# The up products of two MLPs by Strassen's seven half-size products, and attention written out without loops

## The chip, the cores and the metric

The kernel runs on one core of one Trainium2 chip. The metric is device time in microseconds (us) of one launch, lower being better. The kernel before takes 647.9 us, the median of 3 runs (647.8 to 647.93).

## What is computed

The program is an attention block followed by two MLPs. Everything is float32; matrices are multiplied as two float32r parts (a high part and the rest, "hi" and "lo"), three products each: hi·hi, lo·hi and hi·lo.

```
scores = q @ k.T / sqrt(D) + bias(head, distance)      # B=2, H=8, S=768, D=64
keep   = key < n_global  or  0 <= query - key < n_local  # 8 and 96
x  = softmax(where(keep, scores, -1e9)) @ v               # -> 1536 tokens x 512
h  = x @ w_in1;  x2 = (h * sigmoid(h)) @ w_out1           # 512 -> 2048 -> 512
h2 = x2 @ w_in2; y  = (h2 * clip(h2+3, 0, 6) / 6) @ w_out2
```

## The kernel before

**Attention** goes over 8 pairs of heads, 6 query tiles of 128 each: 48 units u. Since a query sees the last 96 keys and 8 global ones, a unit takes 256 columns of keys. For each unit TensorE (PE) makes the scores (L747), turns the probabilities (L756) and multiplies them by the values (L766); VectorE (DVE) adds the bias and finds the row maximum (L427), ScalarE (ACT) makes the exponentials (L596), GpSimd (POOL) normalizes (L301), DVE and ACT share the copies of the turned probabilities (L439, L614), and every third unit ACT and DVE split a group of 384 output columns into `x_hi` and `x_lo` (L619, L444). The pairs run in loops over two pairs (`pairs`), the first and last turn written out.

**The MLPs** work on blocks of 384 tokens (`TB`; `NBLK` = 4 blocks) and chunks of 128 units of the inner width (`FC` = 16). For a chunk PE runs `up` (L849): 4 parts of the depth times 3 terms, 12 matmuls of 384 columns into one of four PSUM banks. In the first MLP ACT takes the sigmoid (L635) and DVE multiplies (L413); in the second DVE does both steps (L566, L570). ACT rounds to `g_hi` (L679), DVE takes the rest, `g_lo` (L542, L575). Then comes `down1` (L864, 12 matmuls of 384 columns) or, in the second MLP, `down2` (L878, 9 matmuls of 512 columns). The order on PE is written by hand: `up` runs two chunks (`AHEAD`) ahead of `down`.

```
for fc in range(FC):
    nxt = fc + AHEAD
    ...
        up(c + AHEAD, FC * mlp + nxt, tb, nxt)
    ...
    down(c, tb, fc, first, last and mlp == 1 and fc == FC - 1)
```

**Weights** stay in SBUF. Each chunk of both matrices (128x1024 in all) comes once per MLP into one of three staging buffers, ACT rounds it to `w_hi` (L641), POOL takes the rest, `w_lo` (L343); both parts then serve all four blocks. Each engine has its own program; the order on each is the order of the code, and semaphores hold it back. SP only issues DMAs.

Of the kernel before, what the change touches and what calls it, by code (L numbers as in the profile page):

```python
# [19 lines left out]
FC = DF // P  # L33
TB = 384
NBLK = NB * S // TB
# [8 lines left out]
STAGES = 3  # L44
LAG = 4
DEEP = 6
AHEAD = 2
# [9 lines left out]
def build(nc, qT, kT, v, w_in1, w_out1, w_in2, w_out2, n_glob, n_loc, out):  # L57
    outer = ExitStack()
    with outer:
# [5 lines left out]

        x_hi = sb("x_hi", [P, 2, NB * KT, TB], F32R)
        x_lo = sb("x_lo", [P, 2, NB * KT, TB], F32R)

        HEAD = 4
        wa_hi = sb("wa_hi", [P, HEAD, 1024], F32R)
        wa_lo = sb("wa_lo", [P, HEAD, 1024], F32R)
        wstage = sb("wstage", [P, STAGES, 1024])
# [5 lines left out]


        attn = ExitStack()
        with attn:
# [3 lines left out]
            with ExitStack() as banded:  # L87
# [12 lines left out]
                m_bias = sb("m_bias", [P, 2, MW], F32, banded)  # L100
                m_tmp = [sb(f"m_tmp{i}", [P, MW], F32, banded) for i in range(5)]
# [10 lines left out]


        gate = sb("gate", [P, 2, TB])
        g_f = sb("g_f", [P, 2, TB])
        g_hi = sb("g_hi", [P, 2, TB], F32R)
        g_lo = sb("g_lo", [P, 2, TB], F32R)
        wb_hi = sb("wb_hi", [P, FC - HEAD, 1024], F32R)
        wb_lo = sb("wb_lo", [P, FC - HEAD, 1024], F32R)
        y_out = sb("y_out", [P, HALF, DM])  # L120
# [5 lines left out]
        def y_bank(i): return ps[:, i, :]  # L126
        def h_bank(c): return ps[:, 4 + c % 4, 0:TB]

        def w_hi(fc): return wa_hi[:, fc, :] if fc < HEAD else wb_hi[:, fc - HEAD, :]
        def w_lo(fc): return wa_lo[:, fc, :] if fc < HEAD else wb_lo[:, fc - HEAD, :]  # L130

        def x_slot(x, it, half):

            return x[:, half, bass.ds(it, 1), :].rearrange("p a t -> p (a t)")

        def x_group(x, j, gm):

# [19 lines left out]
        x_hi_ok = sem("x_hi_ok"); x_lo_ok = sem("x_lo_ok")  # L157
        w_raw = [sem(f"w_raw{i}") for i in range(STAGES)]
        w_hi_ok = sem("w_hi_ok"); w_lo_ok = sem("w_lo_ok")
        h_done = sem("h_done"); gate_ok = sem("gate_ok")  # L160
        g_ok = sem("g_ok"); g_hi_ok = sem("g_hi_ok"); g_lo_ok = sem("g_lo_ok")
        down_done = sem("down_done"); y_hi_ok = sem("y_hi_ok"); y_lo_ok = sem("y_lo_ok")
        relu_ok = sem("relu_ok")
# [3 lines left out]
        a_prt_ok = sem("a_prt_ok"); a_pv = sem("a_pv"); a_xhi = sem("a_xhi"); a_xlo = sem("a_xlo")  # L167
        dve_turn = sem("dve_turn"); pool_turn = sem("pool_turn"); sp_turn = sem("sp_turn")
        y_tile = sem("y_tile"); y_copied = sem("y_copied"); stored = sem("stored")
# [776 lines left out]
```

## Time and profile before

| | |
|---|---|
| median of 3 runs | 647.9 us |
| the profiled execution's own time | 647.83 us |
| its span | 646.1 us |
| PE busy | 627.8 us, 97% |
| DVE / ACT / POOL busy | 260.7 / 208.5 / 128.2 us |
| moved by DMA | 33.16 MB |

The profile is of one execution. Its span runs from the first instruction to the last; the execution's own time is 1.7 us longer. The page gives busy time per engine, the span in 40 slices of about 16 us, and the chain of waits that ended last. A matmul's record lasts until its results are out, so matmuls overlap: the rate is the distance from start to start, not the duration.

### The profile page before, as it was taken

Reading aid. Unit: us, or ns where it says so; the run is one execution under the profiler, and the core shown is the slowest. Engines: PE = TensorE matmul, PEld = TensorE weight load, DVE = VectorE, ACT = ScalarE, POOL = GpSimd, SP = SyncE. Lnnn points to the kernel's source line nnn. Section 1 sums busy time; section 2 is a strip of 40 time slices with the busy share of each in tenths; the row PEclk is TensorE's granted clock in tenths of the full one; section 3 lists DMA queues with packets and bytes.
Section 4 is the critical chain, followed back from the end, with each engine's and each line's share of the span. In section 5 each row is a group of like instructions: output and inputs, shape, how many; then the busy total and the mean of one; then the engine's idle time right before and its main releaser. Section 6 shows DMA issues by size and latency. Waiting matters only on the chain.

```text
span 646.1 us, 10234 instructions
## 1 busy us (share of the span) xinstructions
PE 627.8 (97%) x3600; PEld 566.4 (88%) x3600; DVE 260.7 (40%) x658; ACT 208.5 (32%) x483; POOL 128.2 (20%) x191
## 2 busy tenths in 40 slices
PE   3999998999999999999999999999999999999997
PEld 1555666999999999999999999999999999998996
DVE  4677794322332223222322253443343443343442
ACT  2777875443322223222444431112111111111112
POOL 2656666653000000000255540000000000000000
PEclk9999999999999999999999999999999999999999
DMA  5253643443000000000033300001000100001001
GB/s 197 70 183 112 223 143 132 131 131 97 1 1 2 0 1 0 0 0 0 33 131 125 112 25 0 1 1 49 2 1 0 50 0 0 0 1 50 0 1 49
DMA packets 14872, 33.16 MB, mean 51 GB/s; under 512 B 1904, under 2 KB 2160, under 8 KB 14832
## 3 DMA queue, kind: packets, MB, share of 16 engines
q1 hardware_dynamic: 14832, 32.65, 14.8%
q8 instruction: 23, 0.38, 0.2%
q14 instruction: 17, 0.14, 0.1%
HBM read 29.49 MB, written 3.15 MB: 51 GB/s over the span
## 4 chain that ended last, share of the span: by engine, by line
PE 91%; DVE 3%; issue 2%; ACT 2%; DMA 1%; DVEq 0%; ACTq 0%; POOL 0%; SPq 0%; POOLq 0%
PE ps L849 42%; PE ps L864 21%; PE ps L878 21%; PE ps L747 3%; PE ps L766 3%; PE ps L756 2%; ACT probs L596 1%; DVE negs L427 1%; DMA words<-in_n_loc 1%; DVE probsT L439 1%; ACT m_bias L604 0%; ACT x_hi L619 0%; DVE x_lo L444 0%; DVE g_lo L542 0%; DVE negmax L427 0%
## 5 line engine op out<-in xcount | busy, mean ns | idle before, releaser
L679 ACT ACTIVATE g_hi<-g_f 128x384 fp32r<-128x384 f32 x128 | 67.2, 525 | 332.1 <-PE ps L878 220.2
L849 PE MATMUL ps<-x_hi,wb_hi 128*128 128x384 f32 (+1 forms) x384 | 130.1, 339 | 0.0
L849 PE MATMUL ps<-x_lo,wb_hi 128*128 128x384 f32 (+1 forms) x384 | 130.0, 339 | 0.0
L849 PE MATMUL ps<-x_hi,wb_lo 128*128 128x384 f32 (+1 forms) x384 | 129.8, 338 | 0.0
L542 DVE TENSOR_TENSOR g_lo<-g_f,g_hi 128x384 fp32r<-128x384 f32 x64 | 37.1, 579 | 102.3 <-ACT g_hi L679 99.6
L575 DVE SCALAR_TENSOR_TENSOR g_lo<-g_f,g_hi 128x384 fp32r<-128x384 f32 x64 | 36.4, 568 | 98.1 <-ACT g_hi L679 98.1
L849 PEld LDWEIGHTS ps<-x_hi,wb_hi 128*128 128x128 f32 x384 | 72.0, 188 | 2.1
L849 PEld LDWEIGHTS ps<-x_hi,wb_lo 128*128 128x128 f32 x384 | 72.1, 188 | 2.0
L849 PEld LDWEIGHTS ps<-x_lo,wb_hi 128*128 128x128 f32 x384 | 72.1, 188 | 0.0
L413 DVE TENSOR_TENSOR g_f<-ps,gate 128x384 f32<-128x384 f32 x64 | 35.6, 556 | 84.9 <-ACT gate L635 84.9
L343 POOL TENSOR_TENSOR wb_lo<-wstage,wb_hi 128x1024 fp32r<-128x1024 f32 x24 | 58.1, 2424 | 45.6 <-ACT wb_hi L641 45.5
L864 PE MATMUL ps<-g_hi,wb_hi 128*128 128x384 f32 x192 | 64.8, 338 | 0.0
L864 PE MATMUL ps<-g_hi,wb_lo 128*128 128x384 f32 x192 | 64.6, 336 | 0.0
L864 PE MATMUL ps<-g_lo,wb_hi 128*128 128x384 f32 x192 | 64.4, 336 | 0.0
L566 DVE TENSOR_SCALAR gate<-ps 128x384 f32<-128x384 f32 x64 | 35.7, 557 | 59.4 <-PE ps L849 59.4
L878 PE MATMUL ps<-wb_lo,g_hi 128*128 128x512 f32 x144 | 56.9, 395 | 0.0
L878 PE MATMUL ps<-wb_hi,g_hi 128*128 128x512 f32 x144 | 56.7, 394 | 0.0
L878 PE MATMUL ps<-wb_hi,g_lo 128*128 128x512 f32 x144 | 56.2, 390 | 0.0
L635 ACT ACTIVATE gate<-ps 128x384 f32<-128x384 f32 x64 | 31.4, 491 | 66.5 <-PE ps L849 66.4
L596 ACT ACTIVATE probs<-negs,negmax 128x256 f32<-128x256 f32 (+1 forms) x96 | 46.3, 483 | 18.1 <-DVE negmax L427 17.3
L343 POOL TENSOR_TENSOR wa_lo<-wstage,wa_hi 128x1024 fp32r<-128x1024 f32 x6 | 14.3, 2388 | 169.2 <-ACT wa_hi L641 169.2
L747 PE MATMUL ps<-k_raw,q_raw 64*128 64x256 f32 x192 | 37.0, 467 | 10.5 <-DMA q_raw<-in_qT 8.2
(80 smaller groups left out, 964.9 us busy)
## 6 DMA issues: line engine op xcount, KB each, us to landing
wstage<-in_w_in SPq DMA_DIRECT2D x32, 256.0 KB, 2.6
wstage<-in_w_out SPq DMA_DIRECT2D x32, 256.0 KB, 2.9
v_raw<-in_v SPq DMA_DIRECT2D x8, 704.0 KB, 5.9
k_raw<-in_kT SPq DMA_DIRECT2D x8, 464.0 KB, 3.5
q_raw<-in_qT SPq DMA_DIRECT2D x8, 384.0 KB, 3.9
out_y<-y_out SPq DMA_DIRECT2D x11, 256.0 KB, 2.1
out_y<-y_out SPq DMA_DIRECT2D x2, 128.0 KB, 2.0
words<-in_n_glob SPq DMA_DIRECT2D x1, 1.0 KB, 2.6
```

What stands on the lines that cost most here:

```text
L343: nc.gpsimd.tensor_tensor(w_lo(n % FC), wstage[:, n % STAGES, :], w_hi(n % FC), ALU.subtract).then_inc(w_lo_ok, 1)
L413: nc.vector.tensor_tensor(g_f[:, fc % 2, :], h_bank(fc), gate[:, fc % 2, :], ALU.mult).then_inc(g_ok, 1)
L542: nc.vector.tensor_tensor(g_lo[:, fc % 2, :], g_f[:, fc % 2, :], g_hi[:, fc % 2, :], ALU.subtract).then_inc(g_lo_ok, 1)
L566: nc.vector.tensor_scalar(gate[:, fc % 2, :], h_bank(fc), 3.0, 0.0, ALU.add, ALU.max).then_inc(relu_ok, 1)
L575: nc.vector.scalar_tensor_tensor(g_lo[:, fc % 2, :], g_f[:, fc % 2, :], 1.0 / 6.0, g_hi[:, fc % 2, :], ALU.mult, ALU.subtract).then_inc(g_ ...
L596: nc.scalar.activation(probs[:, um % DEEP, h, a:256], negs[:, um % 2, h, a:256], ACT.Exp, bias=negmax[:, um % DEEP, h:h + 1], scale=-1.0, ...
L635: nc.scalar.activation(gate[:, fc % 2, :], h_bank(fc), ACT.Sigmoid).then_inc(gate_ok, 1)
L679: nc.scalar.activation(g_hi[:, fc % 2, :], g_f[:, fc % 2, :], ACT.Copy, scale=scale).then_inc(g_hi_ok, 1)
L747: mm = nc.tensor.matmul(s_bank(um, h), q_raw[par][D * h:D * h + D, P * t:P * t + P], k_raw[par][D * h:D * h + D, first:first + 256], start ...
L849: mm = nc.tensor.matmul(h, w(fc)[:, P * k:P * k + P], x_blk(x, tb, k), start=(n == 0), stop=(n == len(terms) - 1))
L864: mm = nc.tensor.matmul(y_bank(i)[:, 0:TB], w(fc)[:, a:a + P], g[:, fc % 2, :], start=(fc == 0 and n == 0), stop=(fc == FC - 1 and n == 2))
L878: mm = nc.tensor.matmul(y_bank(i), g[:, fc % 2, P * i:P * i + P], w(fc)[:, 512:1024], start=(fc == 0 and n == 0), stop=(fc == FC - 1 and n ...
```

## The change

Blocks are now 768 tokens (one of the two batches) and steps are 256 units of the inner width: 2 MLPs x 2 blocks x 8 steps (`STEPS`) = 32 steps (`NSTEP`), s = 0 to 31. The 512 x 256 weights of a step and the 512 x 768 tokens are each cut into quarters, and the four quarters of the result are made of seven products (P1 to P7) in place of eight, with sums before and after. A product is 2 parts of the depth times 3 terms, 6 matmuls of 384 columns. PE makes them in the order P1, P2, P6, P5, P7, P3, P4 in two PSUM banks (six others hold the output of the block); P6, P7 and P4 add onto bank 0, P3 onto bank 1. ACT copies P1, P1+P6 and P5 out of PSUM between them (`keep`), DVE adds three of them onto others (`c_sum`).

Weights are no longer kept: in every one of the 32 steps the input weights of a step (`wi_raw`, two buffers) get four sums on POOL (`w_sum`), are rounded on ACT (`w_high`, two halves of 896) and split on DVE (`w_low`); the output weights are rounded on ACT (`wo_high`) and split on POOL. The tokens of a block get four sums on POOL (`x_sum`) and seven quarters split by ACT and DVE (`x_high`, `x_low`, 768 columns each), once per block of each MLP. Attention writes its output unsplit (`x_copy`), has no loops any more, and does the sums and splits of the first two weight steps and of the first block between its units.

```diff
+PRODUCTS = ((A11, B11, 0), (A12, B21, 1), (S2, T2, 0), (S1, T1, 1), (S3, T3, 0), (S4, B22, 1), (A22, T4, 0))
+P1, P2, P6, P5, P7, P3, P4 = range(7)
 # POOL
...
             def banded():
+                for u in range(NU):
+                    total(u)
+                    if u:
+                        norm(u - 1)
+                    if 8 <= u < 16:
+                        w_sum(u // 4 - 2, u % 4)
+                    if 30 <= u < 38 and u % 2 == 0:
+                        x_sum(0, (u - 30) // 2)
+                norm(NU - 1)
...
-            pool.wait_ge(w_lo_ok, AHEAD)
-            for n in range(AHEAD, 2 * FC):
-                pool.wait_ge(w_hi_ok, n + 1)
-                nc.gpsimd.tensor_tensor(w_lo(n % FC), wstage[:, n % STAGES, :], w_hi(n % FC),
-                                        ALU.subtract).then_inc(w_lo_ok, 1)
+            for s in range(NSTEP):
+                pool.wait_ge(wo_hi_ok, s + 1)
+                nc.gpsimd.tensor_tensor(wo_lo[:, s % 2, :], wo_raw[:, s % 2, :], wo_hi[:, s % 2, :],
+                                        ALU.subtract).then_inc(wo_lo_ok, 1)
+                if s + 2 < NSTEP:
+                    for n in range(4):
+                        w_sum(s + 2, n)
+                if s % STEPS == 3 and s < 3 * STEPS:
+                    for n in range(4):
+                        x_sum(s // STEPS + 1, n)
 # DVE
...
+            for s in range(NSTEP):
+                blk, f = s // STEPS, s % STEPS
+                evict = blk > 0 and f == 1
+                mlp2 = s >= NSTEP // 2
+                c_sum(s, 0, 1, p1_c, P2)
+                if mlp2:
+                    hswish(s, 0)
...
+                c_sum(s, 1, 0, p5_c, P7)
+                c_sum(s, 2, 1, u2_c, P3)
...
+                for n in range(1 if mlp2 else 0, 4):
+                    if mlp2:
+                        hswish(s, n)
+                    else:
+                        silu(s, n)
+                g_low(s, 0)
+                g_low(s, 1)
+                if f == STEPS - 1 and s < NSTEP - 1:
+                    for i in range(7):
+                        x_low(blk + 1, i)
+                if s + 2 < NSTEP:
+                    w_low(s + 2, 0)
+                    w_low(s + 2, 1)
 # ACT
...
+            def w_high(s, part):
+
+                at = slice(7 * P * part, 7 * P * part + 7 * P)
+                act.wait_ge(ws_ok, 4 * s + 4)
+                at_least(act, p_done, 7 * (s - 1))
...
+            for s in range(NSTEP):
+                blk, f = s // STEPS, s % STEPS
+                if s:
+                    keep(s, p1_c, 0, P1)
+                keep(s, u2_c, 0, P6)
+                keep(s, p5_c, 1, P5)
...
+                if s < NSTEP // 2:
+                    for n in range(4):
+                        sigmoid(s, n)
+                g_high(s, 0)
+                g_high(s, 1)
+                wo_high(s)
+                if f == STEPS - 1 and s < NSTEP - 1:
+                    for i in range(7):
+                        x_high(blk + 1, i)
+                if s + 2 < NSTEP:
+                    w_high(s + 2, 0)
+                    w_high(s + 2, 1)
 # PE
...
+                elif n == P6:
+                    pe.wait_ge(kept, 3 * s + 1)
+                elif n == P5:
+                    pe.wait_ge(c_ok, 3 * s + 1)
...
+            for s in range(NSTEP):
+                if s and s % STEPS == 0:
+                    down(s - 1, 0)
+                for n in range(2 if s == 0 else 0, 7):
+                    product(s, n)
+                if s and s % STEPS == 0:
+                    down(s - 1, 1)
+                elif s:
+                    if s % STEPS != 0:
+                        down(s - 1, 0)
+                        down(s - 1, 1)
```

The output product keeps its size. Per half of a step (`down1(s, c)`) it is now 12 times a matmul of 512 columns and one of 256; `down2` is 18 matmuls of 512 columns per half. On PE a step is its seven products, then the two halves of `down` of the step before, but at the start of a block (s = 8, 16, 24) one half of `down` goes ahead of the products and the other behind them. At the second step of a block ACT and DVE also copy the finished output of the block before out of PSUM (`y_copy`, 3 pieces each).

On ACT two chunks of the first MLP stood so before, in the block that still rounds weights (`wb_hi` a chunk of weights, `gate` the sigmoid):

```order
L679 ACTIVATE g_hi<-g_f 128x384 [waits down_done,g_ok]
L641 ACTIVATE wb_hi<-wstage 128x1024 [waits w_raw1]
L635 ACTIVATE gate<-ps 128x384 [waits g_ok,h_done]
L679 ACTIVATE g_hi<-g_f 128x384 [waits down_done,g_ok]
L641 ACTIVATE wb_hi<-wstage 128x1024 [waits w_raw2]
```

The rounding of weights waits for nothing but its DMA. In the changed kernel a step of the first MLP stands so on ACT, from the rounding for the step after next to the same place one step on (`ws_ok` counts POOL's sums of weights, `wi_hi` and `wo_hi` are the rounded weights):

```order
L656 ACTIVATE wi_hi<-wi_raw 128x896 [waits p_done,ws_ok] x2
L675 ACTIVATE p1_c<-ps 128x384 [waits c_ok,p_done]
L675 ACTIVATE u2_c<-ps 128x384 [waits c_ok,p_done]
L675 ACTIVATE p5_c<-ps 128x384 [waits c_ok,p_done]
L735 ACTIVATE gate<-c_sb 128x384 [waits g_ok,c_ok] x3
L735 ACTIVATE gate<-ps 128x384 [waits g_ok,p_done]
L741 ACTIVATE g_hi<-g_f 128x768 [waits down_done,g_ok] x2
L724 ACTIVATE wo_hi<-wo_raw 128x1024 [waits down_done,wo_in0]
L656 ACTIVATE wi_hi<-wi_raw 128x896 [waits p_done,ws_ok] x2
```

The copies out of PSUM on which PE's third product waits now stand behind the rounding of weights, which waits for sums on POOL. On POOL a step now is (`wo_hi_ok` counts ACT's rounding of output weights):

```order
L352 TENSOR_TENSOR wo_lo<-wo_raw,wo_hi 128x1024 [waits wo_hi_ok]
L280 TENSOR_TENSOR wi_raw<-wi_raw 128x256 [waits wi_in1]
L282 TENSOR_TENSOR wi_raw<-wi_raw 128x256
L285 TENSOR_TENSOR wi_raw<-wi_raw 128x256 [waits ws_ok]
L288 TENSOR_TENSOR wi_raw<-wi_raw 128x256 [waits ws_ok]
```

The sums thus stand behind a subtraction that waits for the last of ACT's work in the step. Before, POOL had only subtractions of 128x1024, and none after the weights of an MLP were in.

## Rows read from the trace of the kernel before

**Rows 1.** Page, parts 1 and 2: busy time, and 40 slices of 16 us.
```profile
PE 627.8 (97%) x3600; PEld 566.4 (88%) x3600; DVE 260.7 (40%) x658; ACT 208.5 (32%) x483; POOL 128.2 (20%) x191
PEclk9999999999999999999999999999999999999999
```

**Rows 2.** Page, part 4: the chain that ended last, by engine.
```profile
PE 91%; DVE 3%; issue 2%; ACT 2%; DMA 1%; DVEq 0%; ACTq 0%; POOL 0%; SPq 0%; POOLq 0%
```

**Rows 3.** Timeline, first MLP: start us, duration us, engine, line.
```profile
300.40 0.49 ACT L635 ACTIVATE gate<-ps 128x384 f32<-128x384 f32 x1 [1.53 <-PE ps L849]
...
300.93 0.56 DVE L413 TENSOR_TENSOR g_f<-ps,gate 128x384 f32<-128x384 f32 x1 [1.47 <-ACT gate L635]
...
302.31 0.34 PE L849 MATMUL ps<-x_hi,wa_hi 128*128 x1
...
304.40 0.34 PE L864 MATMUL ps<-g_hi,wb_hi 128*128 128x384 f32 x1
```

**Rows 4.** Timeline, second MLP: `down2` from 502.09, `up` from 504.17, `down2` again.
```profile
502.09 0.40 PE L878 MATMUL ps<-wb_hi,g_hi 128*128 128x512 f32 x1
...
504.17 0.34 PE L849 MATMUL ps<-x_hi,wa_hi 128*128 x1
...
506.25 0.39 PE L878 MATMUL ps<-wb_hi,g_hi 128*128 128x512 f32 x1
```

**Rows 5.** Groups by line: busy us, mean ns of one, idle before: ACT.
```profile
L679 ACT ACTIVATE g_hi<-g_f 128x384 fp32r<-128x384 f32 x128 | 67.2, 525 | 332.1 <-PE ps L878 220.2 <-PE ps L864 108.3 <-DVE g_f L413 3.6
L641 ACT ACTIVATE wb_hi<-wstage 128x1024 fp32r<-128x1024 f32 x24 | 25.0, 1046 | 0.0
L604 ACT ACTIVATE m_bias<-m_base,slope 128x384 f32<-128x384 f32 x6 | 3.3, 598 | 0.0
```

**Rows 6.** Timeline, PE: scores at the start of attention and later; eight transposes.
```profile
19.60 1.23 PE L747 MATMUL ps<-k_raw,q_raw 64*128 64x256 f32 x4
...
22.19 0.70 PE L747 MATMUL ps<-k_raw,q_raw 64*128 64x256 f32 x4
...
97.88 1.09 PE L756 MATMUL ps<-ident,probs 128*128 128x128 f32 x8
```

**Rows 7.** Timeline, ACT in attention: two biases back to back.
```profile
53.08 1.11 ACT L604 ACTIVATE m_bias<-m_base,slope 128x384 f32<-128x384 f32 x2
```

**Rows 8.** Groups by line: DVE.
```profile
L542 DVE TENSOR_TENSOR g_lo<-g_f,g_hi 128x384 fp32r<-128x384 f32 x64 | 37.1, 579 | 102.3 <-ACT g_hi L679 99.6 <-issue 2.7
L427 DVE CUSTOM_DVE_ANT_0 negs<-ps,m_bias 128x256 f32<-128x256 f32 x80 | 32.8, 411 | 12.1 <-PE ps L747 6.3 <-ACT probs L596 5.7
L427 DVE CUSTOM_DVE_ANT_0 negs<-ps,m_bias 128x128 f32<-128x128 f32 x16 | 4.4, 280 | 4.9 <-ACT m_bias L604 2.9 <-PE ps L747 2.1
L417 DVE TENSOR_TENSOR wa_lo<-wstage,wa_hi 128x1024 fp32r<-128x1024 f32 x2 | 2.9, 1472 | 0.0
```

**Rows 9.** Timeline near the end of attention: DVE's split, PE's first `up`, POOL.
```profile
94.05 1.47 DVE L417 TENSOR_TENSOR wa_lo<-wstage,wa_hi 128x1024 fp32r<-128x1024 f32 x1
95.00 0.44 PE L849 MATMUL ps<-x_hi,wa_hi 128*128 128x384 f32 x1
95.09 0.47 POOL L292 TENSOR_SCALAR rsume<-rsum 128x2 f32<-128x2 f32 x1 [0.65 <-ACT probs L596]
...
97.24 0.19 POOL L292 TENSOR_SCALAR rsume<-rsum 128x2 f32<-128x2 f32 x1 [0.66 <-ACT probs L596]
```

**Rows 10.** Groups by line: POOL.
```profile
L343 POOL TENSOR_TENSOR wb_lo<-wstage,wb_hi 128x1024 fp32r<-128x1024 f32 x24 | 58.1, 2424 | 45.6 <-ACT wb_hi L641 45.5
```

**Rows 11.** Windows, 30 units of attention: PE, PEld, DVE, ACT, POOL busy; clock; DMA.
```profile
30.79:85.70 54.91, 53.50 (x462) 32.67 (x460) 41.78 (x184) 43.56 (x150) 33.50 (x93) 1.00 0.54 183
```

**Rows 12.** Chain of waits in time: the jump out of attention, the last product.
```profile
105.97 3.15 issue
...
636.70 6.17 PE ps L878 x27
```

More of the change, by code:

```diff
@@ L584, in _, with c_sum @@
-            block2(0, True)
-            with dve.Fori(1, NBLK) as tb:
-                block2(tb, False)
+                for s in range(2):
+                    for part in range(2):
+                        w_low(s, part)
+                for i in range(7):
+                    x_low(0, i)
+            either(dve, banded, general)
+            def c_sum(s, i, bank, add, product):
+                dve.wait_ge(p_done, 7 * s + product + 1)
+                dve.wait_ge(kept, 3 * s + {0: 1, 1: 3, 2: 3}[i])
+                nc.vector.tensor_tensor(c_sb[:, i, :], p_bank(bank), add[:, :], ALU.add).then_inc(c_ok, 1)
@@ L654, in general @@
             def general():
+                act.sem_inc(a_x, 1)
                 with act.Fori(0, NPAIR) as it:
@@ L686, in block1 @@
-            def block1(tb, first, last):
-                for fc in range(FC):
-                    c = FC * tb + fc
-                    if first and fc > 0 and fc + STAGES < FC:
-                        w_high(fc + STAGES)
-                    if not (first and fc == 0):
-                        sigmoid(c, fc)
-                    g_high(c, fc, 1.0)
-                    if fc == AHEAD - 1 and not first:
-                        y_high(tb - 1)
-                    if last and fc >= 2:
-                        w_high(FC + fc - 2)
@@ new lines, in general, with wo_high @@
+                act.wait_ge(a_x, NT * NPAIR + 1)
+                act.sem_inc(x_ok, 2 * NPAIR)
+                for s in range(2):
+                    for part in range(2):
+                        w_high(s, part)
+                for i in range(7):
+                    x_high(0, i)
+                keep(0, p1_c, 0, P1)
+            either(act, banded, general)
+            def wo_high(s):
+                act.wait_ge(wo_in[s % 2], 16 * (s // 2 + 1))
+                at_least(act, down_done, s - 1)
+                nc.scalar.activation(wo_hi[:, s % 2, :], wo_raw[:, s % 2, :], ACT.Copy).then_inc(wo_hi_ok, 1)
@@ L884, in block_ @@
-            def block_(mlp, tb, first, last):
-                down = down1 if mlp == 0 else down2
-                for fc in range(FC):
-                    nxt = fc + AHEAD
-                    c = FC * (NBLK * mlp + tb) + fc
-                    if nxt < FC:
-                        up(c + AHEAD, FC * mlp + nxt, tb, nxt)
-                    elif not last:
-                        up(c + AHEAD, FC * mlp + nxt - FC, tb + 1, nxt - FC)
-                    elif mlp == 0:
-                        up(c + AHEAD, FC + nxt - FC, 0, nxt - FC)
-                    down(c, tb, fc, first, last and mlp == 1 and fc == FC - 1)
```

817 lines of the change are left out of this document (418 added, 399 removed).

## Prediction

> **What bounds the kernel now.** I read the page first. PE is busy 627.8 of 646.1 us, and no slice is below nine tenths of the full clock [rows 1]; the chain that ended last is 91% PE [rows 2]. The other engines have room: DVE 40%, ACT 32%, POOL 20%. So PE sets the time, and the timeline gives its rate. The 12 matmuls of `up` take 304.40 - 302.31 = 2.09 us, 0.174 us each [rows 3]; the 9 matmuls of 512 columns take 504.17 - 502.09 = 2.08 us, 0.231 us each, and the next `up` again 2.08 us [rows 4]. Both are 2.2 columns per ns, so time on PE goes by columns. ACT's `g_high` waited 220.2 + 108.3 us for PE to finish an older `down` [rows 5]: around PE everything is early. A change that takes columns off PE pays until something else is late; the question is what.
>
> **PE's own work.** Per 256 units x 768 tokens `up` had 4 x 12 = 48 matmuls of 384 columns; the seven products have 42. That saves 6 x 0.174 = 1.05 us a step, 33 us in 32 steps. `down2` keeps its columns: 36 x 0.231 = 8.3 us a step. `down1` now alternates 512 and 256 columns. By the rate above 256 columns take 0.116 us; transposes, which load 128 weights for every 128 columns, came every 0.117 us (eight in 1.09, the last of them 0.27 long) [rows 6], so the load does not make it longer. The upper bound is the 0.174 of 384 columns, 1.4 us a step more. I take 0.116: `down1` is 24 x 0.347 = 8.3 us. A step is then 42 x 0.1745 + 8.35 = **15.7 us** of PE, 502 us in all.
>
> **What each operation costs on the other engines.** ACT: 384 columns 0.525 us, 1024 columns 1.046 [rows 5], hence 0.84 for 768 and 0.94 for 896; back to back it starts 0.09 earlier (two biases in 1.11 us where one is 0.598) [rows 5, 7]. DVE: 384 columns 0.56 to 0.58 [rows 3, 8]; from 128 to 256 columns adds 0.131 us, 1.02 ns a column, which makes 896 columns 1.09 us and 768 columns 0.96. The row with 1024 columns, 1.472 us, makes it 1.29 and 1.11 instead [rows 8]. It ran beside POOL's work [rows 9]; in the MLPs POOL will mostly stand idle meanwhile, so I take 1.10 and 0.96 and keep 1.29 and 1.11 for the range. The Trainium skill (VectorE: DVE Perf Modes, on SBUF-source operations) gives (N+151)/0.96 ns for a float32 tensor_tensor, which is 557 ns for 384, as here, and 1224 ns for 1024, where the trace has 1472; by it the sum is the same as by my lower values. POOL: 1024 columns of two inputs 2.42 us; a sum of 256 is between a quarter of that, 0.61, and 0.19 fixed (a 2-column operation) with the rest in proportion, 0.75 [rows 9, 10]. I take 0.70. Passing a result from ACT to DVE costs 300.93 - 300.89 = 0.04 us [rows 3], and I take 0.05 for every pair; a record of PE lasts 0.34 us where the next matmul starts after 0.17, so a product is out 0.2 us after its last slot.
>
> **The new chain.** ACT's order in a step is: three copies out of PSUM, sigmoids, `g_high` x2, `wo_high`, `w_high` for s+2 x2, and only then the copy of P1 of the next step, on which PE's P6 waits. `w_high` waits for POOL's four sums, and those stand behind `wo_lo`, which waits for `wo_high`. DVE has the same: `w_low` x2 ahead of `c_sum` 0, on which P5 waits. So all of it forms one ring, though nothing in s+2's weights is needed soon. Its time, from the start of `wo_lo`:
> `wo_lo` 2.42, four sums 2.9 (one waits for the one before): 5.3. `w_high` first half 0.94 and passing: 6.3. `w_low` 1.03 + 1.10: 8.45. `c_sum` 0 and passing 0.6: 9.1. P5, P7, P3, 18 x 0.1745 and out: 12.4. `c_sum` 2 and three products with the gate, 0.48 + 0.49 + 0.49 + 0.62: 14.5. `g_high` 2 x 0.75: 16.0. `wo_high` 1.05 and passing: **17.1 us**.
> PE has 15.7 us of work in that time, so it stands still 1.4 us in an ordinary step, before P6 and before P5. In the second MLP each gate is two operations on DVE, which adds 0.4 us before the first `g_high` and 0.4 before the second: **17.9 us**, 2.2 us still.
>
> At a block's start the order on PE is other. Between the products of s = 8, 16, 24 and those of the next step lies only one half of `down` (11.5 us with the products), so PE waits 17.1 - 11.5 = 5.6 us there, 6.4 in the second MLP; the copies of finished output add 0.3. At the step before it PE has 15.7 + 4.2 us, more than the ring, and waits for nothing; the 7 x 0.75 = 5.3 us of `x_high` stand in ACT's line where it would have waited 5.3 us for POOL. After step 0 there is no `down` at all: 17.1 - 7.3 = 9.8, of which about 9 show.
>
> **Attention.** ACT gets seven `x_high` and four `w_high`, 7 x 0.84 + 4 x 0.94 = 9.6 us, in 30 units where it is busy 43.6 of 54.9 us: 53.2 then, nearly all. DVE goes from 41.8 to 41.8 - 10 x 0.56 (`x_low` of 384 columns, one in three units) + 4 x 1.10 + 7 x 0.96 = 47.3 [rows 8, 11]. PE is busy 53.5 of 54.9 now, with every unit passing ACT and DVE twice. At best nothing is lost, at worst all that is put on ACT and more, 14 us; I take 8, nearer to ACT's 9.6. The loops' registers and branches go, worth next to nothing where PE does not wait for them. The 2 MB of first weights come in before the third pair: DMA has room at 54% [rows 11].
>
> **Sum.** First product at 95.0 [rows 9] + 8 = 103. The rest of attention inside step 0, with the jump out of it (3.15 us) [rows 12]: 8. PE's work 502. Standing still: first block 9 + 6 x 1.4 = 17.4; second 5.9 + 6 x 1.4 = 14.3; third 6.7 + 6 x 2.2 = 19.9; fourth 6.7 + 5 x 2.2 = 17.7; together 69. From the last matmul to the end 646.1 - 642.9 = 3 us as now [rows 12]. That is a span of 685 us against 646.1. The profiled execution took 1.7 us over its span (647.83, the runs' median 647.9): **687 us**. The 33 us that PE saves are real, and the ring and attention take back 69 + 8, less what no longer fits beside them.
>
> **Rivals.**
> *PE stays the bound* (the other side). It decides whether the ring is under 15.7 us: with POOL's sums at 0.61 (0.4 us less) and 1 us more of overlap between ACT, DVE and POOL than their rows show, ordinary steps would not wait. Then only the four block starts remain, 4.2 to 8 us each, some 20: 103 + 8 + 502 + 20 + 3 + 2 = 638 us. For it: the margin is 1.4 us of 17. Against it: that needs every value at its low end, and the second MLP is 2.2 away. 8%.
> *Contention of DVE and POOL.* POOL's small sum took 0.47 us under DVE's split of weights and 0.19 without it [rows 9]. The ring has ten operations on the two. With DVE's `w_low` at its upper value (2 x 0.19 more), the sums at 0.75 (0.2 more) and `wo_lo` slowed by 0.3 beside `g_low` the ring is 17.1 + 0.9 = 18.0: 32 x 0.9 = 29 us more, 716 us; half of it, 701, is likelier. The Trainium skill (GPSIMD Engine Reference, specifications) says that POOL's SBUF interface is shared with VectorE and contended by DVE instructions with two SBUF inputs; the row agrees, and most of DVE's new operations are of that kind. 17%.
> *PE's clock falls in the gaps.* Scores of one shape took 1.23 us at 19.60 and 0.70 at 22.19 [rows 6]: until then PE ran at the lower of 1.2 and 2.4 GHz, with waits between its groups, though the row of the clock shows nine tenths or more [rows 1]. The new kernel leaves PE idle 5 to 9 us in one piece four times. If the clock falls, the seven products behind the gap take up to 7.3 us more, but those before P6 are done by then: 3 to 7 us four times, 12 to 28 us, 699 to 715. The Trainium skill (TensorE: Matmul & The Clock Gate, on oscillation) says that long enough idle stretches put the clock back to half each time; by it this case happens at four places. 13%.
> *The forecast*, with the ring between 16.6 and 17.6 and attention between 0 and 14: 672 to 703 us. 60%. The last 2% are left for a stall I do not see.
>
> **How the numbers follow.** 687 is the likeliest case. From 664, between the forecast's low end and the PE-bound case, to 716 holds the forecast and nearly all of the two dearer cases; left out are the PE-bound case (8%) and the tails. A measurement of this kernel tells 0.2% (1.3 us) from nothing: faster 0.08, within 0.2% 0.02, slower 0.90.
>
> **What would show it.** In the new profile PE's busy share is near 90% or less; ACT's `wi_hi` waits for POOL's sums (some 5 us a step, 150 in all), DVE's `wi_lo` for `wi_hi`; P6 waits for ACT's copy and P5 for `c_sum`. Starts of P1 lie 17.1 us apart in the first MLP and 17.9 in the second, 11.5 and then 22 at block starts. If steps are 15.7 us apart and PE does not wait, my ring is wrong; if they are further apart with DVE or POOL rows longer than mine, it is contention; if products last twice as long in some slices, it is the clock.

## The result and the profile after

The changed kernel takes 713.25 us (median of 4 runs, 709.41 to 715.55) and the kernel before, run beside it, 647.85. The ratio is 1.1005 [1.095, 1.1061]: 10% slower. The profiled execution took 715.55 us, its span is 713.8. The forecast was 687 (span 685), the range 664 to 716: sign and range hold, and the likeliest value is 26 us too low.

Page of the changed kernel, parts 1, 2, 4 and 5, to be read against [rows 1, 2, 5, 10]:

```profile
PE 626.9 (88%) x3408; PEld 527.8 (74%) x3408; DVE 378.6 (53%) x759; ACT 312.9 (44%) x600; POOL 269.2 (38%) x337
...
PEclk9999979899989998999899998999999999999999
...
PE 27%; POOL 24%; DVE 22%; ACT 14%; issue 13%; DMA 1%; DVEq 0%; ACTq 0%; SPq 0%; POOLq 0%
...
L352 POOL TENSOR_TENSOR wo_lo<-wo_raw,wo_hi 128x1024 fp32r<-128x1024 f32 x32 | 76.7, 2398 | 390.5 <-ACT wo_hi L724 390.5
L850 PE MATMUL ps<-x_hi,wi_hi 128*128 128x384 f32 x448 | 163.4, 365 | 61.6 <-ACT p_c L675 45.2
...
L423 DVE TENSOR_TENSOR wi_lo<-wi_raw,wi_hi 128x896 fp32r<-128x896 f32 x64 | 73.9, 1193 | 170.2 <-ACT wi_hi L656 170.1
```

The chain was 91% PE. Now it goes round through four engines, PE holding 27% of it. PE's busy time has hardly fallen though it has fewer columns to do, since a part of them ran at a lower clock: six digits of the clock's row stand below 9. The waits by line show the ring of the prediction, link by link.

Waits of the changed kernel (total us, times, longest us):

```profile
POOL wo_lo L352 <- ACT wo_hi L724: 390.5, 32, 19.1
DVE wi_lo L423 <- ACT wi_hi L656: 170.1, 28, 6.4
ACT wi_hi L656 <- POOL wi_raw L288: 154.8, 30, 5.4
...
PEld ps L850 <- ACT p_c L675: 54.0, 28, 7.4
...
PE ps L850 <- ACT p_c L675: 45.2, 27, 7.1
```

POOL's 390 us are no loss by themselves: it is an engine with little work that waits. What hurts is ACT's wait for POOL's sum (30 times, 5.2 us each), since ACT's copy of P1 stands behind it, and PE's P6 behind that copy.

One turn of the ring can be read off the timeline of steps 2 and 3 of the first MLP (start, duration, idle before). POOL, then ACT, then DVE, and last PE's P6 in both steps, 16.97 us apart:

```profile
165.95 2.39 POOL L352 TENSOR_TENSOR wo_lo<-wo_raw,wo_hi 128x1024 fp32r<-128x1024 f32 x1 [11.69 <-ACT wo_hi L724]
168.29 0.74 POOL L280 TENSOR_TENSOR wi_raw<-wi_raw 128x256 f32<-128x256 f32 x1
...
170.49 0.73 POOL L288 TENSOR_TENSOR wi_raw<-wi_raw 128x256 f32<-128x256 f32 x1
...
182.91 2.39 POOL L352 TENSOR_TENSOR wo_lo<-wo_raw,wo_hi 128x1024 fp32r<-128x1024 f32 x1 [11.69 <-ACT wo_hi L724]
```

```profile
171.26 1.79 ACT L656 ACTIVATE wi_hi<-wi_raw 128x896 fp32r<-128x896 f32 x2 [5.39 <-POOL wi_raw L288]
172.96 0.47 ACT L675 ACTIVATE p_c<-ps 128x384 f32<-128x384 f32 x1
```

```profile
172.24 2.09 DVE L423 TENSOR_TENSOR wi_lo<-wi_raw,wi_hi 128x896 fp32r<-128x896 f32 x2 [6.20 <-ACT wi_hi L656]
174.25 0.55 DVE L535 TENSOR_TENSOR c_sb<-ps,p_c 128x384 f32<-128x384 f32 x1
...
178.31 0.56 DVE L535 TENSOR_TENSOR c_sb<-ps,u_c 128x384 f32<-128x384 f32 x1 [0.48 <-PE ps L850]
178.78 1.49 DVE L545 TENSOR_TENSOR g_f<-c_sb,gate 128x384 f32<-128x384 f32 x3
```

```profile
156.51 0.44 PE L850 MATMUL ps<-x_hi,wi_hi 128*128 128x384 f32 x1 [0.70 <-ACT p_c L675]
...
173.48 0.44 PE L850 MATMUL ps<-x_hi,wi_hi 128*128 128x384 f32 x1 [0.70 <-ACT p_c L675]
```

From one `wo_lo` to the next: 182.91 - 165.95 = **16.96 us**. The prediction's 17.1 was made link by link, and so it can be held against these rows: weights' sums done after 5.3 us (5.31 here, 171.26 - 165.95), `w_low` done after 8.45 (8.38, 174.33), `c_sum` 2 at 12.4 (12.36), the next `wo_lo` at 17.1.

The starts of P1 in the timeline of PE give the whole sum. A step s runs here from its P1 to the next one:

```
                            forecast   measured   difference
first product               103        110.54      +7.5
step 0                       15.3       18.23      +2.9
step 1                       24.7       24.77      +0.1
8 ordinary steps, MLP 1      17.1 each  16.88-16.98 -1.1
9 ordinary steps, MLP 2      17.9 each  17.56-17.64 -2.6
steps 4, 12, 20           17.1/17.1/17.9  21.9/21.76/21.34 +12.9
steps 7 to 9, 15 to 17, 23 to 25  54.4/55.2/56.0  57.3/57.7/58.7 +8.1
step 31 and the end          27.0       27.3       +0.3
span                         685.6      713.8     +28.2
```

The forecast column is the prediction's own terms laid out step by step (a step's 15.7 us of PE plus its standing still; where a block starts, 19.9, 11.5 and 15.7 us of PE for the three steps). The ring, on which the sign rested, was right within 2%. Three other entries make the error: the steps in which POOL also sums tokens, the block starts, and attention.

**Steps 4, 12, 20.** In steps 3, 11 and 19 POOL does the four sums of the next block's tokens right behind those of the weights. Timeline of POOL, then of DVE, for step 3:

```profile
188.15 1.84 POOL L301 TENSOR_TENSOR x_t<-x_raw 128x768 f32<-128x768 f32 x1
190.07 2.55 POOL L304 TENSOR_TENSOR x_t<-x_raw,x_t 128x768 f32<-128x768 f32 x1
192.58 2.66 POOL L306 TENSOR_TENSOR x_t<-x_raw 128x768 f32<-128x768 f32 x1
195.20 1.82 POOL L309 TENSOR_TENSOR x_t<-x_raw,x_t 128x768 f32<-128x768 f32 x1
```

```profile
189.21 4.36 DVE L423 TENSOR_TENSOR wi_lo<-wi_raw,wi_hi 128x896 fp32r<-128x896 f32 x2 [6.20 <-ACT wi_hi L656]
193.49 0.54 DVE L535 TENSOR_TENSOR c_sb<-ps,p_c 128x384 f32<-128x384 f32 x1
```

Next to POOL's two-input sums, `w_low` takes 4.36 us for two instead of 2.09, and POOL's sums 2.55 and 2.66 instead of 1.84. So P5 comes 2.3 us late (idle 2.33 us before it), and inside that gap, at 193.1, PE's granted clock falls (windows: us, busy of PE, PEld, DVE, ACT, POOL, granted clock, DMA share, GB/s):

```profile
187.00:193.00 6.00, 4.06 (x22) 3.37 (x20) 3.79 (x2) 2.66 (x4) 5.84 (x5) 1.00 0.16 59
193.00:200.00 7.00, 5.91 (x19) 5.91 (x20) 1.59 (x3) 1.43 (x3) 4.02 (x2) 0.51 0.24 75
```

The 18 matmuls of P5, P7 and P3 behind it take 6.06 us to their last result, instead of the 3.41 of step 3: at 0.51 of full clock, the lower of 1.2 and 2.4 GHz. 2.3 + 2.65 = 4.9 us, the whole excess over the 16.97 of its neighbours.

**Block starts.** Timeline of POOL and of DVE in step 7: seven splits `x_low` on DVE meet POOL's sums of weights.

```profile
258.06 1.48 POOL L280 TENSOR_TENSOR wi_raw<-wi_raw 128x256 f32<-128x256 f32 x1
```

```profile
256.40 3.96 DVE L432 TENSOR_TENSOR x_lo<-x_raw,x_hi 128x768 fp32r<-128x768 f32 x2 [0.59 <-ACT x_hi L669]
260.28 4.32 DVE L432 TENSOR_TENSOR x_lo<-x_t,x_hi 128x768 fp32r<-128x768 f32 x3
264.53 0.94 DVE L432 TENSOR_TENSOR x_lo<-x_raw,x_hi 128x768 fp32r<-128x768 f32 x1
```

A small sum takes 1.48 us where it takes 0.74 alone, a split 1.98 and 1.44 where 0.94 is its own time. `w_low` then starts late, and P5 of step 8 waits 1.12 us. In step 9 the matmuls behind PE's longest gap of the block (4.80 us before P6) run mostly at the half clock: the 30 from P6 to P4 take 7.44 us to their last result, against 5.4 at 0.174 each.

**Attention.** PE's clock falls there too, 90.7 us from the start. PE had stood idle 1.07 and 1.48 us before its groups of `values` at 83.82 and 88.98, but experiment 3 will show the same idle times without a fall (windows as above):

```profile
85.00:90.00 5.00, 3.52 (x34) 2.27 (x32) 2.92 (x11) 4.20 (x12) 3.96 (x8) 1.00 0.00 2
90.00:95.00 5.00, 4.44 (x26) 2.43 (x22) 4.18 (x18) 4.40 (x15) 3.87 (x8) 0.57 0.34 90
95.00:100.00 5.00, 5.00 (x25) 2.97 (x24) 2.77 (x11) 1.75 (x7) 2.97 (x6) 0.50 0.69 267
```

At half clock PE itself is the late engine for 10 us. What that costs is read under experiment 3.

### The profile page after: what moved, and what is told of

Read it like the earlier page. It is cut to its first block, busy times and chain, and to the rows that moved or that the text cites. A ratio compares the mean times of both kernels' runs of the same rounds, so it can differ in the third digit from the quotient of the medians.

```text
span 713.8 us, 9497 instructions
## 1 busy us (share of the span) xinstructions
PE 626.9 (88%) x3408; PEld 527.8 (74%) x3408; DVE 378.6 (53%) x759; ACT 312.9 (44%) x600; POOL 269.2 (38%) x337
## 2 busy tenths in 40 slices
DMA packets 14883, 50.08 MB, mean 70 GB/s; under 512 B 1904, under 2 KB 2160, under 8 KB 14832
## 4 chain that ended last, share of the span: by engine, by line
PE 27%; POOL 24%; DVE 22%; ACT 14%; issue 13%; DMA 1%; DVEq 0%; ACTq 0%; SPq 0%; POOLq 0%
PE ps L850 19%; POOL wo_lo L352 9%; DVE wi_lo L423 6%; DVE x_lo L432 4%; ACT wo_hi L724 4%; ACT wi_hi L656 4%; PE ps L922 4%; POOL wi_raw L288 3%; POOL wi_raw L285 3%; DVE g_f L545 3%; POOL wi_raw L280 3%; POOL wi_raw L282 3%; DVE gate L554 2%; ACT probs L626 2%; DVE c_sb L535 2%
## 5 line engine op out<-in xcount | busy, mean ns | idle before, releaser
L352 POOL TENSOR_TENSOR wo_lo<-wo_raw,wo_hi 128x1024 fp32r<-128x1024 f32 x32 | 76.7, 2398 | 390.5 <-ACT wo_hi L724 390.5
L850 PE MATMUL ps<-x_hi,wi_hi 128*128 128x384 f32 x448 | 163.4, 365 | 61.6 <-ACT p_c L675 45.2
L850 PE MATMUL ps<-x_hi,wi_lo 128*128 128x384 f32 x448 | 156.5, 349 | 0.0
L850 PE MATMUL ps<-x_lo,wi_hi 128*128 128x384 f32 x448 | 156.1, 348 | 0.0
L850 PEld LDWEIGHTS ps<-x_hi,wi_hi 128*128 128x128 f32 x448 | 89.0, 199 | 80.6 <-ACT p_c L675 54.0
L850 PEld LDWEIGHTS ps<-x_hi,wi_lo 128*128 128x128 f32 x448 | 89.2, 199 | 0.6
L850 PEld LDWEIGHTS ps<-x_lo,wi_hi 128*128 128x128 f32 x448 | 88.9, 198 | 0.0
L922 PE MATMUL ps<-wo_hi,g_lo 128*128 128x512 f32 x192 | 76.5, 399 | 0.0
L922 PE MATMUL ps<-wo_hi,g_hi 128*128 128x512 f32 x192 | 75.5, 393 | 0.8 <-DVE y_out L581 0.4
L922 PE MATMUL ps<-wo_lo,g_hi 128*128 128x512 f32 x192 | 75.7, 394 | 0.0
```

Of the source, the lines that this page charges most:

```text
L352: nc.gpsimd.tensor_tensor(wo_lo[:, s % 2, :], wo_raw[:, s % 2, :], wo_hi[:, s % 2, :], ALU.subtract).then_inc(wo_lo_ok, 1)
L850: mm = nc.tensor.matmul(p_bank(bank), w[:, s % 2, at], x[:, b, k, :], start=fresh and k == 0 and i == 0, stop=k == 1 and i == 2, skip_grou ...
L922: mm = nc.tensor.matmul(y_bank(t), g[:, s % 2, c, P * t:P * t + P], wo[:, s % 2, DM * c:DM * c + DM], start=s % STEPS == 0 and c == 0 and ...
```

## The experiments

Each kernel was timed beside the kernel before on the same chip, whose median was 647.9 to 648.0 each time. The theory after the result: (A) the ring sets the ordinary step; (B) DVE and POOL slow each other when both run two-input operations, and that makes steps 4, 12, 20 and part of the block starts; (C) the clock falls in some of the gaps and charges for it; (D) attention is dear because the work put there has no cover. The rival to A is that a step is dear whatever the order, by the number of operations alone. The larger DMA traffic (50.08 MB, before 33.16) is no rival: in the MLPs of the changed kernel no wait is put down to a DMA.

### 1. The rounding of weights out of the ring

```diff
                 keep(s, p5_c, 1, P5)
+                if s and s + 1 < NSTEP:
+                    w_high(s + 1, 0)
+                    w_high(s + 1, 1)
...
-                if s + 2 < NSTEP:
-                    w_high(s + 2, 0)
-                    w_high(s + 2, 1)
```

and on DVE `w_low(s + 1, ...)` in the same way behind `g_low(s, 1)`.

> The rounding and splitting of the input weights stands one step later on ACT and DVE: w_high(s+1) behind the three copies of step s, w_low(s+1) behind g_low of step s. Everything else is as in the changed kernel, the sums on POOL too. If the ring (copy of P1 behind w_high behind POOL's sums behind wo_high) sets the steps, ordinary steps fall from 17.0 and 17.6 us to PE's own 15.7 in both MLPs, the gaps at block starts of 5 to 7 us nearly go, and with them the stretches of low clock in the MLPs: 713 - 13 x 1.3 - 14 x 1.9 - 4 x 6 - some 20 of clock and contention, about 625 to 645 us. If what counts is contention of DVE and POOL alone, ordinary steps stay at 17.0 and 17.6 us. If the clock falls whatever the gaps are, steps stay uneven and the time is over 670.

Measured: 671.93 us, ratio 1.0386 [1.036, 1.0413]. Undisturbed steps are 15.64 us apart in the first MLP and 16.04 in the second: A holds, and the products' saving is real. But the total is 27 us above the upper end of what was expected, for `w_low` now runs beside `wo_lo`. Some 34 us at the half clock are left too (mean 0.975); how much of the 27 us is theirs was not separated. Page, part 1, DVE's timeline around step 4, and POOL's beside its second row:

```profile
PE 613.4 (92%) x3408; PEld 524.2 (78%) x3408; DVE 441.9 (66%) x759; ACT 309.0 (46%) x600; POOL 314.9 (47%) x337
```

```profile
185.37 4.17 DVE L545 TENSOR_TENSOR g_f<-c_sb,gate 128x384 f32<-128x384 f32 x3
...
192.19 4.26 DVE L423 TENSOR_TENSOR wi_lo<-wi_raw,wi_hi 128x896 fp32r<-128x896 f32 x2
```

```profile
192.18 3.33 POOL L352 TENSOR_TENSOR wo_lo<-wo_raw,wo_hi 128x1024 fp32r<-128x1024 f32 x1 [3.53 <-ACT wo_hi L724]
```

The same 759 operations occupy DVE 63 us longer than in the changed kernel, and POOL's 337 46 us longer. In eight steps P1 then waits for `w_low`, 20.9 us in all. B holds wherever the two meet, not only at the token sums: beside those, three products with the gate take 4.17 us, where they take 1.49 alone.

### 2. Token sums apart, one a step

```diff
             for s in range(NSTEP):
+                if s % STEPS >= 4 and s < 3 * STEPS:
+                    pool.wait_ge(c_ok, 3 * s + 1)
+                    x_sum(s // STEPS + 1, s % STEPS - 4)
                 pool.wait_ge(wo_hi_ok, s + 1)
...
-                if s % STEPS == 3 and s < 3 * STEPS:
-                    for n in range(4):
-                        x_sum(s // STEPS + 1, n)
```

> The four sums of a block's tokens on POOL are spread over the last four steps of the block before (one each, behind a wait for the first c_sum), so that they run while DVE waits for P7 and not beside w_low. Contention theory: w_low in the fourth step of a block goes from 2.2 us apiece back to 1.1, that step's stretch from 21.9 to 17.0 us, three times: about 14 us less, 696 to 702. If the long step came from POOL's queue being full and not from DVE being slowed, it would shorten too, but DVE's w_low would have shown 1.1 us before; if it came from neither, nothing changes.

Measured: 702.17 us, ratio 1.0838 [1.0792, 1.0885], 11 us under the changed kernel. Steps 4, 12 and 20 take 16.99, 16.97 and 17.64 us, like their neighbours. Timelines of DVE and of POOL, whose first token sum now stands behind its wait in step 4:

```profile
189.49 2.09 DVE L423 TENSOR_TENSOR wi_lo<-wi_raw,wi_hi 128x896 fp32r<-128x896 f32 x2 [6.22 <-ACT wi_hi L656]
```

```profile
192.13 1.85 POOL L301 TENSOR_TENSOR x_t<-x_raw 128x768 f32<-128x768 f32 x1 [3.66 <-DVE c_sb L535]
```

Same operations, same count, another time: 2.09 for 4.36, and every token sum of a block now takes 1.8 to 2.0 us, where the two in the middle took 2.55 and 2.66. What the three steps cost was the meeting (with the fall of the clock in its gap), not the work. They give back 13.4 us together; the second steps of the blocks grew by 2.0 together, which was not followed.

### 3. PE kept busy in its longest gap

```diff
                 for n in range(2 if s == 0 else 0, 7):
+                    if s == 1 and n == P6:
+                        for _ in range(48):
+                            nc.tensor.transpose(y_bank(4)[:, 0:P], ident[:, :], ident[:, :])
                     product(s, n)
```

The transposes go to a PSUM bank that is idle then, and compute nothing that is used.

> 48 transposes of the identity into an idle PSUM bank stand on PE between P2 and P6 of step 1, where PE was idle for 7.1 us; they compute nothing. Clock theory: PE stays at work there, the clock does not fall behind this gap, and the first products of step 1 and down(0) run at the full rate: the stretch from step 1 to step 2 goes from 24.8 to about 23.7 us, the time falls by 1 to 4 us. If the gap has nothing to do with the clock, that stretch stays at 24.8 or grows by what the transposes take beyond the gap.

Measured: 708.65 us (707.44 to 709.86), ratio 1.0938. Windows of the changed kernel, then of this one, over step 1 and over the end of attention:

```profile
128.77:153.54 24.77, 17.66 (x90) 16.34 (x91) 9.20 (x13) 9.51 (x15) 9.59 (x10) 0.86 0.18 56
85.00:106.00 21.00, 18.97 (x128) 11.32 (x128) 14.23 (x54) 15.09 (x48) 12.83 (x27) 0.76 0.25 85
```

```profile
124.28:147.77 23.49, 21.48 (x138) 19.89 (x139) 9.21 (x13) 9.51 (x15) 9.63 (x10) 1.00 0.17 56
85.00:106.00 21.00, 17.13 (x153) 10.41 (x149) 16.42 (x61) 17.79 (x56) 15.54 (x34) 1.00 0.25 85
```

With PE busy in the gap, all but the last 1.94 us before P6, the clock stays at its upper level in step 1, which takes 23.49 us instead of 24.77: the fall at this place (6.8 us at the half clock) costs 1.3 us. That is less than the 2.65 us of step 4. The second pair of rows shows something that was not sought. Up to 106 us both kernels run the same instructions, yet here the clock did not fall in attention, and the first product starts at 105.99 instead of 110.54. The fall in attention thus cost 4.6 us of the 7.5 by which the forecast missed there. Six profiled executions have these same instructions in attention without a change, and bear it out: with 10.2 us at the half clock there (the changed kernel, experiments 1, 2 and 6) the first product starts at 110.5 to 110.8, without (experiments 3 and 5) at 105.9 to 106.0. What decides whether the clock falls is open, for PE's idle times ahead of that place are the same (timeline of PE, the changed kernel, then this one):

```profile
88.98 0.66 PE L822 MATMUL ps<-probsT,v_raw 128*64 128x128 f32 x8 [1.48 <-DVE probsT L454]
```

```profile
88.14 0.66 PE L822 MATMUL ps<-probsT,v_raw 128*64 128x128 f32 x8 [1.47 <-DVE probsT L454]
```

The other runs of the changed kernel point the same way: mean clocks of 0.962 and 0.964 go with 715.55 and 715.01 us, 0.973 and 0.974 with 709.41 and 711.5.

### 4. The first block's token work behind attention

The four token sums, `x_high`, `x_low` and P1, P2 of step 0 move behind the last unit (POOL shown; ACT, DVE and PE in the same way):

```diff
-                    if 30 <= u < 38 and u % 2 == 0:
-                        x_sum(0, (u - 30) // 2)
                 norm(NU - 1)
+                for n in range(4):
+                    x_sum(0, n)
```

> The sums and splits of block 0's tokens are taken out of attention and stand behind it (P1 and P2 of step 0 too). If they are what slowed attention (ACT and DVE full from unit 33 on), the scores of the last unit start near 96 us in place of 106, as before the change (93.4); the time then shows whether it is cheaper behind: four sums of 1.9 us on POOL and seven splits in a row cost 8 to 12 us there, so 709 to 716 in all. If the slow units come from the weights' sums or from the clock, the last unit stays at 103 or later and the time grows by 8 or more.

Measured: 710.21 us, ratio 1.0962. The last unit's scores start at 97.9 instead of 106.5 (93.41 in the kernel before). Not all of these 8.6 us are the moved work's: this execution has no fall of the clock in attention, and without a fall the unmoved work gives 101.9 (experiments 3 and 5). So the token work slows attention by 4.0 us, and the fall by the other 4.6. Taken out, the work is as dear: P1 starts at 110.64, 4.7 us later than without a fall (105.9), for without units beside it `x_low` is what PE waits for (2.97 us). Step 0 is shorter by 4.8 us (13.4) and step 1 longer by 1.1 (25.84). D is half right: the work costs about the same on either side.

### 5. Only DVE's part of the order moved

```diff
                 c_sum(s, 2, 1, u2_c, P3)
+                if s and s + 1 < NSTEP:
+                    w_low(s + 1, 0)
+                    w_low(s + 1, 1)
```

(and its old place removed; ACT keeps its order)

> Only DVE's part is moved: w_low(s+1) stands behind the third c_sum of step s, no longer at the end of step s-1; ACT's w_high(s+2) stays where the change put it. DVE has the same work and fewer waits in front of c_sum 0. By a theory of load or contention this is no slower than the change. By the ring theory it is slower: the ring no longer passes w_low before c_sum 0 (2.1 us less, of which P6's wait for the copy gives back 1.6), but it passes w_low between P3 and the gates, so 2.4 us more: ordinary steps 18.7 us in the first MLP and 19.5 in the second against 17.0 and 17.6, about 740 to 760 in all.

Measured: 776.34 us, ratio 1.1968 [1.1904, 1.2032]. `w_low` now stands in the ring between `c_sum` 2 and the products with the gate, behind work of PE, instead of beside it. Two ordinary steps of the first MLP ran without a fall of the clock, in 18.61 and 18.63 us, close to the 18.7 that A gives (a third, behind the 28.8 us of step 9, took 15.6); steps with a fall take 20.2 us, and those of the second MLP mostly 20.6. The total lies above the expectation, since the mean clock is 0.929. A gap of one length did not always bring a fall: P6 waits as long in step 2 (18.61 us) as in step 3 (20.17 us), and only in step 3 is a matmul's record 0.68 us long (timeline of PE):

```profile
155.37 0.45 PE L850 MATMUL ps<-x_hi,wi_hi 128*128 128x384 f32 x1 [2.70 <-ACT p_c L675]
...
173.98 0.68 PE L850 MATMUL ps<-x_hi,wi_hi 128*128 128x384 f32 x1 [2.69 <-ACT p_c L675]
```

The rival to A is out: the same operations give 15.6, 17.0 or 18.6 us a step, by their order alone.

### 6. Both orders and the spread sums together

Experiment 1 with `w_low(s + 1)` where experiment 5 has it, and POOL as in experiment 2.

> e1 with two more moves: w_low(s+1) behind the third c_sum of step s (when POOL stands idle) in place of behind g_low, and the sums of tokens spread as in e2. Ring and contention theory: ordinary steps 15.7 us in both MLPs, no long step where the block's tokens are summed (17.3 to 18.9 in e1), the two stretches at a block's start 12 to 14 and 16 to 19 us in place of 17 and 20; PE's clock falls less often. 672 - 11 (sums of tokens) - 12 to 20 (block starts) = 640 to 650 us. If w_low at the end of a step was not what held the block starts up in e1, they stay at 17 and 20 and the time is about 660.

Measured: 648.05 us (10 runs, 645.35 to 650.68), ratio 0.9991 [0.9971, 1.0012]. Page, part 1:

```profile
PE 604.2 (93%) x3408; PEld 518.3 (80%) x3408; DVE 380.7 (59%) x759; ACT 309.0 (48%) x600; POOL 267.0 (41%) x337
```

DVE's and POOL's busy times are back at 381 and 267, and the time is 24 us under experiment 1. In the MLPs the two engines now meet only ahead of a block start, where sums and `x_low` still take up to 1.46 and 2.54 us. Ordinary steps are 15.63 and 15.71, the forecast's own work of PE. What is left over the kernel before is, in the main, attention (first product 110.84, before 95.0 [rows 9]) and the second step of each block: 19.29, 21.48 and 21.31 us. There PE waits before `down` for a copy of finished output (timeline of PE in step 9):

```profile
266.93 0.47 PE L913 MATMUL ps<-g_hi,wo_hi 128*128 128x512 f32 x1 [3.36 <-DVE x_raw L581]
```

### 7. Step 1's weights out of attention

```diff
-                    if 8 <= u < 16:
+                    if 8 <= u < 12:
                         w_sum(u // 4 - 2, u % 4)
...
-                if s and s + 1 < NSTEP:
+                if s + 1 < NSTEP:
                     w_low(s + 1, 0)
```

> e6, and the sums, rounding and splitting of step 1's input weights are taken out of attention into step 0, as every later step has them. If the weights' work slowed attention (units 17 to 25, 4.6 us between the last unit of e4 and that of the kernel before), the first product comes 2 to 3 us earlier; step 0 gets longer by up to 2 us, since POOL does the sums behind attention. 0 to 3 us faster than e6. If POOL's sums in a row hold up step 1, it is 1 to 3 us slower.

Measured: 650.35 us, ratio 1.0034 [1.0011, 1.0056], 2.3 us more than experiment 6. The first product starts 4.8 us earlier (106.03), and steps 0 and 1 give back 3.2 and 1.2 (21.57, 17.26). But the earlier start is not the moved weights' doing: this execution had no fall of the clock in attention before 104.7 us, and experiments 3 and 5, with the weights still there, start at 105.99 and 105.94 without one. So the move gained nothing that can be seen in attention, and cost 4.4 us in steps 0 and 1. The rest of the profiled difference of 3.0 us is in the second steps of the blocks, 3.3 us together; 2.5 of it in step 9, where the clock fell for 6.8 us and had not fallen in experiment 6. The expectation failed: the weights of step 1 are better where they were.

### 8. Finished output ahead of the ring

```diff
+                out_now = blk > 0 and f == 1
+                if out_now:
+                    y_copy(blk - 1, 0)
                 if s:
                     keep(s, p1_c, 0, P1)
+                if out_now:
+                    y_copy(blk - 1, 2)
                 keep(s, u2_c, 0, P6)
```

and so on for the other pieces, on DVE around `c_sum` 0; the three behind the copies are gone. The rest is experiment 6.

> e6, and at the second step of a block the six copies of finished output go first: on ACT between the copies of P1, P1+P6 and P5, on DVE around the first c_sum, all before the weights. In e6 down of that step waited for copies that stood behind w_high and w_low. If so, the stretches of 19.3, 21.5 and 21.3 us become 16 to 17 (PE's own is 15.7), 3 x 3 to 5 us less with fewer falls of the clock: 648 - 9 to 13 = 635 to 640 us, under the kernel before (648). If those stretches are long for another cause (products waiting for tokens, the clock), they stay over 19 and the time is 647.

Measured: 632.7 us, ratio 0.9769 [0.975, 0.9788], 15 us under experiment 6. The second steps of blocks fall from 19.29, 21.48 and 21.31 to 16.08, 16.65 and 16.65: 12.7 us from a reordering of six copies. Another 2.4 us come from an earlier first product (108.41), behind 6.8 us at the half clock in attention instead of 10.2, and are not the copies' doing. The prediction had set these copies at 0.3 us. In the ring that was so (PE waited 0.4 us for them in each of the three places); as soon as the ring is cut they are what `down` waits for.

### 9. Half of the first block's token work behind attention

Experiment 8, with two of the four sums, and three of seven `x_high` and `x_low`, moved into step 0.

> e8, and of block 0's tokens only two sums and four splits are done in attention, one in four units; the other two sums and three splits stand in step 0, where ACT, DVE and POOL are mostly idle. If ACT's and DVE's load in units 33 to 47 slows attention and lets the clock fall there, the first product comes at 103 to 106 us in place of 111 and step 0 is 1 to 2 us longer: 2 to 6 us less than e8. If attention was held up by something else, the first product stays at 110 and the time is 0 to 2 us over e8.

Measured: 629.26 us (627.61 to 630.01), ratio **0.971 [0.969, 0.9729]**. Page, part 1:

```profile
PE 596.9 (95%) x3408; PEld 514.1 (82%) x3408; DVE 381.4 (61%) x759; ACT 309.0 (49%) x600; POOL 263.7 (42%) x337
```

The first product starts at 102.43, and step 0 takes 19.24 (18.66 in experiment 8, from 108.41). The clock did not fall in attention here, so that of these 6.0 us 3.5 are left for the moved work, against the 105.9 of executions without a fall. This version beats both kernels: 18.7 us under the kernel before, 84 under the changed one, with the same products and the same number of operations.

## Why the prediction was right, and where it was not

**PE's own work, 15.7 us a step: right.** Steps of 15.63 and 15.71 us in experiments 6, 8 and 9. `down1` with its alternating 512 and 256 columns keeps its time, as taken: the 256 columns take 0.12 us from start to start (152.73 to 152.85 in the timeline), not the upper bound of 0.174.

**The ring: right, and shown.** 16.97 for 17.1, 17.64 for 17.9. Breaking it gave 15.6 (experiment 1), lengthening it 18.6 (experiment 5). Link by link the rows of the first MLP stay within 0.15 us of the forecast; in which link the second MLP's 0.26 us lie was not looked at. One sentence of the prediction is wrong where its sum is right: in the step before a block start PE was to wait for nothing, yet the sum has 1.4 or 2.2 us for steps 7, 15 and 23. PE stood still there as elsewhere (0.70 us before P6 in step 7), and these steps took 21.1, 21.1 and 21.8 us against 19.9 of work.

**The operations' lengths: right where they run alone.** `w_low` 1.05 to 1.09 each (taken 1.10, upper 1.29), `x_low` 0.94 (0.96), sums 0.74 (0.70, upper bound 0.75).

**The token sums on POOL: the step that failed.** The part on the new chain does not name them at all, so that they stand in the sum at nothing. As work on an idle POOL they are nothing. They run beside `w_low`, which is in the ring, and the three steps lay 12.9 us above the forecast; experiment 2 made them 13.4 us shorter, and the whole 11. The rival of contention had the mechanism and the wrong place. It put small supplements on every step (0.9 us), while undisturbed steps show none, because in the ring DVE and POOL take turns; the cost falls, doubled, on the few steps where they meet.

The Trainium skill (GPSIMD Engine Reference, specifications) names two SBUF inputs on DVE as a case of contention. The rows agree (2.09 against 4.36 us for one pair), and they add the size, which was the thing missing.

**Block starts: mechanism right, size off.** 5.9 and 6.7 us of standing still were taken for each; measured is 2.5 to 2.9 more. That `x_high` stands where ACT would have waited for POOL holds for ACT (its wait for sums falls from 5.39 to 3.05 us), but `x_low` beside the sums makes sums 1.45 us and splits 1.4 on average (seven in 9.9). At the first of the three starts the rows divide the 2.9: step 8 took 1.4 us more than its 11.5, with P5 waiting behind the late `x_low` (12.87 in experiments 6 and 8 too, which have no ring), and step 9 took 1.7 more, where the half clock lengthened 30 matmuls by 2.0; step 7 took 0.2 less.

**The clock: a rival at 13%, and partly true.** It was to fall at four places and cost 12 to 28 us. The mean clock of 0.962 over 713.8 us amounts to 54 us at the half level, in nine stretches: at the block starts, in the first steps, at the 2.3 us gaps of steps 4, 12 and 20, and in attention. Where it was measured the price is less than half the length, since PE has waits to absorb it: 1.3 us at step 1, 2.65 us at step 4, 4.6 in attention. The cases had been laid out as excluding each other. They came together: contention makes gaps, and in gaps the clock fell. So the result is at the upper end of the range. That it still lies inside is partly luck: the bound of 716 stood for a ring of 18.0 us in every step, which no undisturbed step showed (16.97 and 17.64); other terms filled the room.

**Attention +8: measured +15.5.** Of the 7.5 that were missed 4.6 are the clock. The rest, 2.9, is within the 0 to 14 that was given for the engines' load. Step 0 was 2.9 longer than its term; 3.4 us at the half clock lie in it, which can make at most half of that length, and the rest was not followed.

## What to carry to other kernels

Before an algorithm that saves matmuls is given to a kernel bound by PE, follow each in-order engine once round: work for a later step that waits for another engine, and stands ahead of what PE needs now, makes a ring whose length replaces PE's work as the step time. Place such work behind the last thing that PE waits for, and let two-input operations of DVE and POOL take turns. When several risks share a cause (a gap that also lowers the clock), price them together and not as alternatives.

## What the runs showed that was not expected

- Two-input operations on float32 in SBUF on DVE and POOL at once slow both: DVE's 896 columns from 1.05 to 2.18 us (half of a pair), POOL's 256 columns from 0.74 to 1.48, its 768 from 1.84 to 2.66. Over a whole kernel that made 61 us of DVE's busy time (441.9 against 380.7, experiments 1 and 6).
- The granted clock went from 1.00 to about half in single gaps of 2.3 us between products, and in attention behind idle times of 1.07 and 1.48 us within 6 us. It did not always do so: not in attention in two executions of the same instructions with the same idle times, and not in one of two gaps of 2.7 us (experiment 5). Four runs of the changed kernel differ by 6 us; four of the kernel before, timed beside them, by 0.6, and 19 of it in a later series by 3.4.
- Order outweighed the count of operations: with the same products and the same operations, the order alone spans 629 to 776 us.
